# Network columns in the attention's order, accumulators opened by transposes, and probabilities times values in four groups per pair

## The reference

```python
# attention: q, k, v (2, 8, 768, 64); a key counts only where its hash bucket is the query's
mask = q_bucket[:, :, :, None] == k_bucket[:, :, None, :]
scores = np.where(mask, scale * np.matmul(q, k.transpose(0, 1, 3, 2)), -1e9)
attn = np.exp(scores - max); attn = attn / (sum + 1e-09); x = attn @ v      # x: (2, 768, 512)
# network: x plus the real part of the 2-D Fourier transform over sequence and features
u = x + np.real(np.fft.fft(np.fft.fft(x, axis=1), axis=2))
un = (u - mean) / np.sqrt(var + 1e-6)
x2 = u + np.maximum(un @ w_ch1, 0.0) @ w_ch2                                 # 512 -> 2048 -> 512
# gate: a causal convolution of 5 taps over the sequence
gate = sigmoid(sum(conv_w[k] * shifted(x2, 4 - k) for k in range(5)))
out = (gate * (x2 @ w_val)) @ w_out
```

## Time and profile before

| | |
|---|---|
| time, median of 3 runs | 663.28 us (663.13 to 665.55) |
| the profiled execution's own time | 663.62 us |
| its span in the trace | 661.8 us |
| TensorE matmuls busy | 634.2 us (96%), 3810 records |
| VectorE busy | 353.8 us (53%) |
| ScalarE busy | 317.0 us (48%) |
| POOL busy | 245.4 us (37%) |
| chain that ended last | TensorE 84%, VectorE 8%, issue 3%, POOL 2% |

### The profile page before, as it was taken

The page is one execution under the profiler, slowest core; times in us unless marked ns, Lnnn a source line. Parts: engine busy times, 40 slices in busy tenths (PEclk is TensorE's granted clock), DMA queues, the critical chain, the costliest instruction groups (busy, mean ns, idle before and its releaser), DMA issues.

```text
span 661.8 us, 11290 instructions
## 1 busy us (share of the span) xinstructions
PE 634.2 (96%) x3810; PEld 508.4 (77%) x3810; DVE 353.8 (53%) x585; ACT 317.0 (48%) x606; POOL 245.4 (37%) x201
## 2 busy tenths in 40 slices
PE   2999999999999999889999999999999999999998
PEld 1667676767666675888888888889888888888786
DVE  2978786968787785987211111115433333329920
ACT  2877776868686765364322222224333333255242
POOL 6643333333252440845333222235544444313140
PEclk9999999999999999999999999999999999999999
DMA  5922231314241000100122222431212222000102
GB/s 127 247 77 72 72 95 48 95 48 108 59 119 57 15 25 1 49 0 1 33 65 63 63 63 63 141 115 33 63 63 63 63 63 63 16 1 1 64 32 95
DMA packets 34263, 42.08 MB, mean 64 GB/s; under 512 B 3521, under 2 KB 22209, under 8 KB 34241
## 3 DMA queue, kind: packets, MB, share of 16 engines
q1 hardware_dynamic: 32512, 37.77, 19.7%
q0 software_dynamic: 1728, 4.02, 2.3%
HBM read 38.63 MB, written 3.15 MB: 63 GB/s over the span
## 4 chain that ended last, share of the span: by engine, by line
PE 84%; DVE 8%; issue 3%; POOL 2%; ACT 1%; DMA 1%; SPq 0%; DVEq 0%; ACTq 0%
PE banks L1516 20%; PE banks L1504 20%; PE banks L1319 10%; PE banks L1302 10%; PE banks L1366 7%; PE banks L1595 4%; PE banks L1611 4%; DVE row_min L970 2%; PE banks L1258 2%; PE banks L1439 2%; PE banks L1491 1%; DVE probT L342 1%; DVE k_b L963 1%; PE banks L1342 1%; POOL row_sums_and_differences L540 1%
## 5 line engine op out<-in xcount | busy, mean ns | idle before, releaser
L1165 DVE SCALAR_TENSOR_TENSOR h_lo<-banks,h_hi 128x512 fp32r<-128x512 f32 x64 | 35.5, 558 | 186.4 <-ACT h_hi L826 186.4
L970 DVE TENSOR_REDUCE row_min<-banks 128x1 f32<-128x768 f32 x96 | 91.3, 956 | 44.3 <-PE banks L1302 43.8
L677 ACT ACTIVATE prob<-banks,row_min 128x768 f32<-128x768 f32 x96 | 87.0, 906 | 30.1 <-DVE row_min L970 30.1
L1504 PE MATMUL banks<-unT_hi,w_hi 128*128 128x512 f32 (+1 forms) x256 | 86.5, 338 | 0.0
L1504 PE MATMUL banks<-unT_hi,w_lo 128*128 128x512 f32 (+1 forms) x256 | 86.3, 337 | 0.0
L1504 PE MATMUL banks<-unT_lo,w_hi 128*128 128x512 f32 (+1 forms) x256 | 86.2, 337 | 0.0
L1366 PE MATMUL banks<-ident,prob 128*128 128x128 f32 x576 | 79.7, 274 | 2.2 <-DVE probT L342 1.2
L563 POOL TENSOR_TENSOR w_lo<-w_stage,w_hi 128x512 fp32r<-128x512 f32 x32 | 45.1, 1411 | 83.2 <-ACT w_hi L742 83.2
L1366 PEld LDWEIGHTS banks<-ident,prob 128*128 128x128 f32 x576 | 67.2, 140 | 10.2 <-ACT probT L342 2.6
L501 POOL TENSOR_TENSOR k_b<-k_raw,k_a 64x768 fp32r<-64x768 f32 x16 | 29.2, 1823 | 123.2 <-ACT k_a L660 123.2
L1319 PE MATMUL banks<-probT,v_in 128*64 128x384 f32 x384 | 72.3, 498 | 0.7 <-ACT outT L687 0.7
(11 more groups left out here) (149 smaller groups left out, 1204.1 us busy)
## 6 DMA issues: line engine op xcount, KB each, us to landing
w_stage<-in_moe_w_ch SPq DMA_DIRECT2D x64, 256.0 KB, 2.8
q_raw<-in_q SPq DMA_DIRECT2D x32, 192.0 KB, 3.3
k_raw<-in_k SPq DMA_DIRECT2D x32, 192.0 KB, 3.6
v_in<-in_v SPq DMA_DIRECT2D x16, 192.0 KB, 2.4
out<-y_out SPq DMA_DIRECT2D x12, 256.0 KB, 2.0
seq_tables_sb<-in_dft POOLq DMA_DIRECT2D x6, 386.0 KB, 3.6
wvo_stage<-in_moe_w_val SPq DMA_DIRECT2D x1, 1024.0 KB, 5.4
wvo_stage<-in_moe_w_out SPq DMA_DIRECT2D x1, 1024.0 KB, 7.9
```

The lines of the kernel that those rows point to most:

```text
L677: act.activation(prob[s % 2][:, :, :], s_tile(s), ACT.Exp, bias=row_min[:, s:s + 1], scale=-1.0, accum_out=row_sum[:, s:s + 1]).then_inc(e ...
L970: dve.tensor_reduce(row_min[:, s:s + 1], s_tile(s), AX.XY, ALU.min).then_inc(min_ready, 1)
L1165: dve.scalar_tensor_tensor(out=h_lo[:, slot, at:at + size], in0=h_bank[c], scalar=0.0, in1=h_hi[:, slot, at:at + size].bitcast(F32), op0=A ...
L1504: op = pe.matmul(h_bank[c], w_[:, slot, kb, :], x_[:, kb, at:at + size], start=(kb == 0 and m == 0), stop=(kb == KB - 1 and m == 2))
```

## The change

Three things are changed. The normalised, transposed network inputs are written in the attention's order, as they come, and so are the hidden products and the accumulators; `natural` is gone, and the copies out of the accumulators (`take_x2`) restore natural order, with four copies per block instead of three, two of them reversed. The accumulators are opened by transposes (`is_transpose=True`) of whole tiles with the identity: per block four in the first chunk and two in the second, where there were five and three f32 matmuls; the matrix `reverse` and its two instructions on POOL are gone. And `PV_SLOTS` has four groups of six matmuls per pair, in slots 11, 1, 2 and 4, in place of six groups of four. The numbers of the semaphores follow.

```diff
--- before.py
+++ after.py
@@ -60,7 +60,6 @@
-        reverse = sb("reverse", [P, P])
@@ -238,7 +237,7 @@
-        PV_SLOTS = {11: (0, 0), 0: (0, 1), 1: (0, 2), 2: (1, 0), 3: (1, 1), 4: (1, 2)}
+        PV_SLOTS = {11: (0, 0), 1: (0, 1), 2: (1, 0), 4: (1, 1)}
@@ -382,19 +381,6 @@
-        def unT_pieces(n):
-
-            return n + 1 + n // T + (n % T >= ORDER.index(HT))
-
-        def natural(t):
-
-            if t < HT:
-                return [(slice(0, P), slice(t * P, (t + 1) * P))]
-            first = S - (t - HT) * P
-            if t == HT:
-                return [(slice(1, P), slice(first - 1, first - P, -1)), (slice(0, 1), slice(S // 2, S // 2 + 1))]
-            return [(slice(0, P), slice(first, first - P, -1))]
...
@@ -755,8 +738,7 @@
                 act.wait_ge(un_transposed, n + 1)
                 src = PS[:, un_bank(n), :].rearrange("p (k m) -> p k m", k=KB)
-                for rows, cols in natural(t):
-                    act.copy(un_hi[b][:, :, cols], src[:, :, rows]).then_inc(unT_hi_done, 1)
+                act.copy(un_hi[b][:, :, t * P:(t + 1) * P], src).then_inc(unT_hi_done, 1)
...
@@ -834,10 +816,11 @@
                     half = x2[b][:, 2 * d + 1, PAD:PAD + HALF]
-                    act.copy(half[:, 0:C0 - HALF], PS[:, d, HALF:C0]).then_inc(x2_by_act, 1)
-                    act.copy(half[:, C0 - HALF:HALF], acc(d, 1)).then_inc(x2_by_act, 1)
-                act.wait_ge(x2_by_act, 6 * (b + 1))
-                act.wait_ge(x2_by_dve, 6 * (b + 1))
+                    act.copy(half[:, 0:1], PS[:, d, HALF:HALF + 1]).then_inc(x2_by_act, 1)
+                    act.copy(half[:, C1 + 1:HALF], PS[:, d, C0 - 1:HALF:-1]).then_inc(x2_by_act, 1)
+                    act.copy(half[:, C1:0:-1], acc(d, 1)).then_inc(x2_by_act, 1)
+                act.wait_ge(x2_by_act, 8 * (b + 1))
+                act.wait_ge(x2_by_dve, 8 * (b + 1))
...
@@ -1314,11 +1297,11 @@
-                for kt in (2 * part, 2 * part + 1):
+                for kt in range(HT * part, HT * part + HT):
                     for h in range(2):
                         op = pe.matmul(PS[h * D:(h + 1) * D, 7, 0:HALF], v_in[:, h, kt, :],
                                        probT[h][:, kt, g * HALF:(g + 1) * HALF], start=(kt == 0), stop=(kt == T - 1))
-                if part == 2:
+                if part == 1:
                     op.then_inc(pv_done, 1)
...
@@ -1474,23 +1457,11 @@
             def open_acc(b, d, c):
 
-                low, high = c * C0, (C0, S)[c]
-                first = c == 0 or d % 2 == 0
-                for t in range(T):
-                    for rows, cols in natural(t):
...
-                        pe.matmul(acc(d, c)[:, left - low:right - low], X[:, b, t, d * P:(d + 1) * P],
-                                  mover[:, at:at + right - left], start=first, stop=False, skip_group_check=True)
-                        first = False
+                tiles = (range(C0 // P), range(C0 // P, T))[c]
+                for t in tiles:
+                    at = t * P - c * C0
+                    pe.matmul(acc(d, c)[:, at:at + P], X[:, b, t, d * P:(d + 1) * P], ident[:, :], is_transpose=True,
+                              start=(t == tiles[0] and (c == 0 or d % 2 == 0)), stop=False, skip_group_check=True)
```

More of the change, by code:

```diff
@@ L481, in _ @@
             pool.memset(ident[:, :], 0.0).then_inc(consts_ready, 1)
-            pool.memset(reverse[:, :], 0.0).then_inc(consts_ready, 1)
-            pool.wait_ge(consts_ready, 7)
-            pool.affine_select(out=reverse[:, :], in_=reverse[:, :], compare_op=ALU.not_equal, fill=1.0,
-                               base=1 - P, pattern=[[1, P]], channel_multiplier=1).then_inc(consts_ready, 1)
+            pool.wait_ge(consts_ready, 6)
             pool.affine_select(out=ident[:, :], in_=ident[:, :], compare_op=ALU.not_equal, fill=1.0,
@@ L507, in split_qk @@
                     .then_inc(lo_done, 1)
-            pool.wait_ge(consts_ready, 9)
+            pool.wait_ge(consts_ready, 7)
             scale_q(0, 0)
@@ L613, in finish_x2 @@
             def finish_x2(b):
[L614 to L615 removed]
+                pool.wait_ge(x2_by_act, 8 * (b + 1))
+                pool.wait_ge(x2_by_dve, 8 * (b + 1))
                 pool.tensor_copy(x2[b][:, 1:2 * KB:2, 0:PAD], x2[b][:, 0:2 * KB:2, HALF:HALF + PAD])\
@@ L1078, in unT_lo @@
                 b, t = tile_at(n)
-                pieces = natural(t)
-                dve.wait_ge(unT_hi_done, unT_pieces(n))
+                dve.wait_ge(unT_hi_done, n + 1)
                 src = PS[:, un_bank(n), :].rearrange("p (k m) -> p k m", k=KB)
-                for rows, cols in pieces:
-                    dve.tensor_tensor(un_lo[b][:, :, cols], src[:, :, rows], un_hi[b][:, :, cols].bitcast(F32),
-                                      ALU.subtract).then_inc(unT_lo_done, 1)
+                cols = slice(t * P, (t + 1) * P)
+                dve.tensor_tensor(un_lo[b][:, :, cols], src, un_hi[b][:, :, cols].bitcast(F32),
+                                  ALU.subtract).then_inc(unT_lo_done, 1)
             def cos_and_sin(step):
@@ L1188, in take_x2 @@
                     half = x2[b][:, 2 * d + 1, PAD:PAD + HALF]
-                    dve.tensor_copy(half[:, 0:C0 - HALF], PS[:, d, HALF:C0]).then_inc(x2_by_dve, 1)
-                    dve.tensor_copy(half[:, C0 - HALF:HALF], acc(d, 1)).then_inc(x2_by_dve, 1)
+                    dve.tensor_copy(half[:, 0:1], PS[:, d, HALF:HALF + 1]).then_inc(x2_by_dve, 1)
+                    dve.tensor_copy(half[:, C1 + 1:HALF], PS[:, d, C0 - 1:HALF:-1]).then_inc(x2_by_dve, 1)
+                    dve.tensor_copy(half[:, C1:0:-1], acc(d, 1)).then_inc(x2_by_dve, 1)
             dve.wait_ge(taps_spread, 2)
@@ L1196, in _ @@
             take_x2(0)
-            dve.wait_ge(x2_by_act, 6)
+            dve.wait_ge(x2_by_act, 8)
             dve.wait_ge(x2_lead, B + 1)
@@ L1410, in transpose_un @@
                 if before is not None:
-                    pe.wait_ge(unT_lo_done, unT_pieces(before))
+                    pe.wait_ge(unT_lo_done, before + 1)
                 for kb in range(KB):
@@ L1475, in open_acc @@
             def open_acc(b, d, c):
-                low, high = c * C0, (C0, S)[c]
-                first = c == 0 or d % 2 == 0
-                for t in range(T):
-                    for rows, cols in natural(t):
-                        if cols.step == -1:
-                            left, right = max(cols.stop + 1, low), min(cols.start + 1, high)
-                            base = S - (t - HT) * P - (P - 1)
-                            mover, at = reverse, left - base
-                        else:
-                            left, right = max(cols.start, low), min(cols.stop, high)
-                            mover, at = (reverse, P - 1) if rows.stop == 1 else (ident, left - cols.start)
-                        if left >= right:
-                            continue
-                        pe.matmul(acc(d, c)[:, left - low:right - low], X[:, b, t, d * P:(d + 1) * P],
-                                  mover[:, at:at + right - left], start=first, stop=False, skip_group_check=True)
-                        first = False
+                tiles = (range(C0 // P), range(C0 // P, T))[c]
[3 more added lines that the diff above has]
+                              start=(t == tiles[0] and (c == 0 or d % 2 == 0)), stop=False, skip_group_check=True)
             def ffn1(n, b, slot):
@@ L1559, in _ @@
             ffn1(FB, 1, 0)
-            pe.wait_ge(x2_by_act, 6)
-            pe.wait_ge(x2_by_dve, 6)
+            pe.wait_ge(x2_by_act, 8)
+            pe.wait_ge(x2_by_dve, 8)
             for d in range(KB):
@@ L1582, in values @@
                     if d == 1:
-                        pe.wait_ge(x2_by_act, 12)
+                        pe.wait_ge(x2_by_act, 16)
                     if d == 2:
-                        pe.wait_ge(x2_by_dve, 12)
+                        pe.wait_ge(x2_by_dve, 16)
                 elif d == 0:
```

18 lines of the change are left out of this document (8 added, 10 removed).

## The result

The changed kernel takes 654.95 us (median of 4, 654.22 to 655.48) against 663.25 for the kernel before beside it; the ratio is 0.9865, 95% interval 0.9846 to 0.9883. Forecast was 653.5. The profiled execution took 655.48, its span is 653.7, and it is the longest of the four. Its mean granted clock is 0.995; over the four executions it is 0.995, 1.000, 0.997 and 0.995, in the order 655.48, 654.22, 655.21, 654.69.

What follows compares the result with a forecast made beforehand. TensorE, busy 96% of the span, was taken as the bound. Savings of 4.5 + 4.05 + 1.5 - 0.2 = 9.85 us took the profiled 663.62 to 653.8, or 653.5 against the median; range 652.0 to 657.0.

Steps and rivals of the forecast that it cites:

- the forecast's own case: Whole kernel: the predicted savings hold as summed, time 652.5 to 654.7 us, chance 0.70.
- The PV groups: Attention's probabilities-times-values matmuls: two group edges fewer save 0.6 us per pair of heads, 4.5 us in all.
- (a): Attention: group edges worth only their ends, 0.3, or VectorE's half takes part back; attention brings 2.2, time 655.8; chance 0.12.
- (b): Attention brings nothing, since ACT or VectorE sets the period; time 658.0 us; chance 0.05.
- rival (e): Attention slot 1: TensorE arrives before slot 11's exponential, each pair shows a minimum-exponential chain; time 668.1 us; chance 0.02.
- Second opening: Second batch's accumulators: 24 one-record transposes replace 32 f32 matmuls, 7.06 to 2.65 us; 4.05 saved after a wait.
- Rival (c): Accumulator openings: an accumulation-starting transpose costs two records; second batch's takes 5.3 us, 3.2 less saved, time 656.7; chance 0.04.
- First opening: First batch's accumulators: fewer records by transposes, and no split of the mirrored tile; 1.5 us saved (1.0 to 2.0).
- the single pieces: First batch: the mirrored tile's small extra pieces on ScalarE and VectorE go, 0.25 us saved (0 to 0.6).
- The x2 copies: Copies out of the accumulators: four per block instead of three, the new one a single column; cost 0.2 us (0 to 0.5).
- the last of the sum: Whole-kernel total: profiled execution lies 0.34 us above the median of three runs, so 653.8 becomes 653.5.
- Rival (d): Behind the second batch's accumulator opening: TensorE's clock falls to half, 2.7 to 6.9 us lost, time 656.2 to 660.4; chance 0.03.

## Why the prediction was right, and where it was off

654.95 lies inside the range, 1.45 above the forecast and 0.25 above the upper end of the forecast's own case; but the mechanisms are those of that case. Step by step:

- **The PV groups** were forecast at 0.6 a pair and 4.5 in all. The period went from 30.69 to 30.01, 0.68. TensorE reached the transforms 4.43 earlier, but the profiled execution had also started 0.38 later; from the first pair's slot 11 on it is 4.81 (226.69 less 221.88), 0.3 above the forecast. The medians, with clock and start in them, say 4.1 for undoing it and 4.2 for doing it alone. The reasoning is borne out: the price of an edge read from the earlier trace rows (a group of 12 records takes 2.09 from 98.40 to 100.49 and one of 24 takes 4.02 in the run with two groups, 0.161 a record and again 0.16 fixed), and the slots laid out one by one. The light half is 11.24 long before and after. Rivals (a) and (b) fall.
- **Where rival (e) sat.** Its mechanism, TensorE too early for an exponential in slot 1, isn't there: the margin was 1.0 as computed. But the threat behind it is real, one step further. With one group less, VectorE's minima and copies set the pace, and the sign turns. I had named VectorE as the limit of slots 5 to 10 with 10.36 of 11.24 busy; what I had not seen is that the group in slot 4 keeps that figure from growing.
- **Second opening:** 4.05 forecast, 4.10 measured; 24 records in 2.78 (2.65 forecast), the wait behind it 0.18 (0.3). Rival (c), two records for a transpose, falls; with f32 matmuls, which do take two, the stretch is 5.28 where the rival said 5.3.
- **First opening:** 1.5 forecast. From the first opening to the product behind it 11.04 (308.56 to 319.60) became 9.83 at full clock, so 1.21, and the transforms ahead of it gained 0.1 (263.13 to 303.82 became 258.25 to 298.84 in that same profile). Together 1.3, 0.2 less than forecast; no run separates the 1.25 for the opening from the 0.25 for the single pieces. With f32 matmuls of whole tiles there it is 10.13, so the columns' order is worth 0.9 and the record saved only 0.3 here: the wait for ScalarE's and VectorE's parts takes the rest.
- **The x2 copies:** 0.2 forecast, 0.15 measured between the values and the end (0.09 to 0.17 with other pairs of traces). Mirrored copies cost what straight ones do on VectorE, within 4 ns, and some 20 ns more on ScalarE, where the four copies of one form differ by some 50. I had given the mirroring no price, from ScalarE's pieces. These are ScalarE's and VectorE's mirrored copies in the changed kernel,

```profile
L821 ACT COPY x2T<-banks 128x256 f32<-128x256 f32 x4 | 1.7, 430 | 0.0
L820 ACT COPY x2T<-banks 128x127 f32<-128x127 f32 x4 | 1.2, 309 | 0.0
...
L1173 DVE COPY x2T<-banks 128x256 f32<-128x256 f32 x4 | 1.6, 412 | 0.0
L1172 DVE COPY x2T<-banks 128x127 f32<-128x127 f32 x4 | 1.1, 278 | 0.0
```

and these the straight ones of 256 and 128 columns in the kernel before:

```profile
L838 ACT COPY x2T<-banks 128x256 f32<-128x256 f32 x4 | 1.6, 409 | 0.0
L837 ACT COPY x2T<-banks 128x128 f32<-128x128 f32 x4 | 1.2, 290 | 0.0
...
L1190 DVE COPY x2T<-banks 128x256 f32<-128x256 f32 x4 | 1.7, 416 | 0.0
L1189 DVE COPY x2T<-banks 128x128 f32<-128x128 f32 x4 | 1.1, 282 | 0.0
```

- **The step that was off** is the last of the sum: from the profiled execution's own time to the median. I read "the granted clock is full in every slice" as a property of the kernel. It is one of that execution, and besides, a row that prints 9 from 90% up can hide a stretch at half. Of the 1.68 us between the sum of 9.85 and the 8.17 of the two profiles, 1.5 is the lower clock level (1.32 in the feature products, 0.19 in the first opening) and 0.38 the later start; the first opening was forecast 0.2 too high, attention 0.3 too low. At full clock the changed kernel takes 653.75 in the median of only three executions (652.98 to 654.22), 9.6 less than the kernel before at full clock (663.38). There was also a draw in the result that I had no hold on: three of the changed kernel's four executions have the lower level, while three of the four beside it of the kernel before, by their times of 663.13 to 663.28, don't. Four executions at full clock would have given about 653.75, four others about 655.28; that the median lies 1.45 above the forecast, and not 0.25 or 1.8, is luck.
- **Rival (d)** named the lower clock level, but behind the second opening, where the granted clock is 1.00 in every profile. The rule that I weighed (transposes don't count as work for the clock; the Trainium skill, TensorE: Matmul & The Clock Gate, Part 4: PE-mode transpose) is not shown at work by any run here: 24 transposes in a row at 450.33 are followed by a granted clock of 1.00, and 10 us of nothing but transposes and waits, from 303.15 to 313.41, ran at 1.00 too. Some part of the transposes in the lower level of the first opening isn't excluded.

## What to carry to other kernels

Price a group's edge by two groups of different length in the same trace, then lay the new slots out one by one and compare each with the engine that has to follow: a long group on the busiest engine is also a pause in which the second busiest catches up, and its place can be worth more (1.3 us a pair for the one in slot 4) than its edges (0.3). Read the clock and the time of every execution, not the profiled one's alone, before a sum is anchored to a median: here 17 of 39 executions of the same kernel had a lower mean clock, and their median is 1.75 us longer. And compare stages from a common point inside the run: the start alone differed by up to 1.9 us between profiles. And where the lower clock level shows up behind a wait of TensorE, a few matmuls without a use put into that wait can be worth trying: with 14 of them the changed kernel took 653.80 with a spread of 0.4 us, beside 654.95 and 654.52 without (the ratios to the kernel before, 0.9841 from 0.9826 to 0.9855 and 0.9859 from 0.9839 to 0.9880, still overlap). In the kernel before the same 14 kept the clock full and gained nothing that the median shows: 663.86 beside 663.60.

## What the runs showed of the hardware

TensorE's clock went to its lower level (0.50 and 0.51 granted, 1.2 GHz) in some executions and not in others of the same program. In two profiles this came shortly behind a wait of 1.7 us, and in three in a stretch of transposes with waits of about 1 us between them; the wait of 1.73 us is there in the profile at full clock too. In the feature products it cost 1.3 us of the stage, and in the first opening, where TensorE waits for ScalarE anyway, 0.2, 0.3 and 0.9. Filling that one wait with matmuls kept the clock full in all 22 executions; filling half of it kept it in four of five. What decides an execution stays open.

A copy of one column from PSUM lasts 147 ns on VectorE and 191 on ScalarE, but its neighbour starts 0.05 to 0.07 us behind it. With one such copy more for each block, two blocks on each engine, and two of the others reversed, the stretch from the values to the end grew by 0.15 us.
